# A fused attention and mixing kernel: one exponential, two folds and a division change places at the end of the attention stage

## What is computed

```
def phi(x):
    proj = np.einsum('bhsd,df->bhsf', x, w_phi)
    proj = proj - np.max(np.abs(proj), axis=-1, keepdims=True)
    return np.concatenate([np.exp(proj), np.exp(-proj)], axis=-1)
q_p, k_p = (phi(q), phi(k))
kv = np.einsum('bhsf,bhsd->bhfd', k_p, v)
z = np.sum(k_p, axis=2)
num = np.einsum('bhsf,bhfd->bhsd', q_p, kv)
den = np.einsum('bhsf,bhf->bhs', q_p, z)[..., None] + 1e-06
return (num / den).astype(np.float32)
```

```
X = np.fft.fft(x, axis=1)
X = np.fft.fft(X, axis=2)
mixed = np.real(X).astype(np.float32)
u = x + mixed
...
ch = np.maximum(un @ w_ch1, 0.0) @ w_ch2
return (u + ch).astype(np.float32)
```

## Time and profile before

| | |
|---|---|
| time, median of 3 (lowest to highest) | 1013.8 us (1013.75 to 1014.8) |
| time of the profiled execution | 1013.84 us |
| its span, first to last instruction | 1012.0 us |
| mean granted clock of TensorE | 0.989 of full |
| busy: TensorE / VectorE / ScalarE / GpSimd | 1001.8 / 654.7 / 557.3 / 364.6 us |
| attention and transform, until the perceptron has TensorE alone | about 272 us |

### The profile page before, as it was taken

How to read it: one execution, slowest core, us unless ns; L and a number is a source line. 1 busy time by engine, 2 the same in 40 slices (tenths; PEclk the granted TensorE clock), 3 DMA queues, 4 the chain that set the end, 5 groups by cost and what they waited for, 6 DMA issues and landing times.

```text
span 1012.0 us, 16785 instructions
## 1 busy us (share of the span) xinstructions
PE 1001.8 (99%) x5866; PEld 928.5 (92%) x5866; DVE 654.7 (65%) x1156; ACT 557.3 (55%) x1018; POOL 364.6 (36%) x362
## 2 busy tenths in 40 slices
PE   9999999998999999999999999999999999999997
PEld 8999999998999899899999998999999999989996
DVE  6676769887875567565675556846567455765443
ACT  5655555753575555555656656556655566634431
POOL 3633334533252444413533236323272242622110
PEclk9999999996999999999999999999999999999999
DMA  6333132201153223232232331332324322242202
GB/s 181 72 92 90 38 72 54 54 13 33 58 151 105 63 67 105 66 99 83 64 94 67 90 104 45 91 95 69 99 63 136 104 67 90 63 141 67 63 2 63
DMA packets 101313, 80.31 MB, mean 79 GB/s; under 512 B 56944, under 2 KB 81776, under 8 KB 101232
## 3 DMA queue, kind: packets, MB, share of 16 engines
q1 hardware_dynamic: 100992, 78.91, 28.0%
q10 hardware_dynamic: 240, 0.33, 0.1%
HBM read 66.10 MB, written 4.72 MB: 70 GB/s over the span
## 4 chain that ended last, share of the span: by engine, by line
PE 95%; DVE 3%; issue 1%; ACT 0%; DVEq 0%; ACTq 0%
PE bank L1180 39%; PE bank L1157 35%; PE bank L408 6%; PE bank L421 5%; PE bank L374 3%; PE bank L660 2%; PE bank L680 2%; PE bank L392 1%; PE bank L426 1%; PE bank L368 1%; DVE shift_k L483 0%; DVE xall L544 0%; PE bank L331 0%; DVE amax_k L470 0%; DVE xn L1515 0%
## 5 line engine op out<-in xcount | busy, mean ns | idle before, releaser
L1180 PE MATMUL bank<-w2op,hid 128*128 128x512 f32 x1728 | 423.2, 390 | 0.0
L1180 PEld LDWEIGHTS bank<-w2op,hid 128*128 128x128 f32 x1728 | 321.6, 188 | 53.4 <-issue 0.3
L1157 PE MATMUL bank<-x_T,w1op 128*128 128x384 f32 x1152 | 208.1, 335 | 0.0
L1157 PEld LDWEIGHTS bank<-x_T,w1op 128*128 128x128 f32 x1152 | 201.2, 188 | 3.9
L1157 PE MATMUL bank<-x_B,w1op 128*128 128x384 f32 x864 | 173.5, 336 | 0.0
L1157 PEld LDWEIGHTS bank<-x_B,w1op 128*128 128x128 f32 x864 | 154.4, 188 | 11.4
L1351 POOL TENSOR_TENSOR w_sums<-st_w 128x256 f32<-128x256 f32 x48 | 49.3, 1028 | 224.4 <-DVE w1op L1387 224.4
L1467 DVE SCALAR_TENSOR_TENSOR hid<-part_s,hid 128x384 fp32r<-128x384 f32 x141 | 98.2, 723 | 37.7 <-ACT hid L1463 37.6
L1408 DVE TENSOR_TENSOR w2op<-st_w,w2op 128x1024 fp32r<-128x1024 f32 x48 | 62.7, 1306 | 45.9 <-ACT w2op L1404 45.9
L1319 POOL TENSOR_TENSOR x_sums<-xraw 128x256 f32<-128x256 f32 x30 | 22.3, 764 | 194.5 <-ACT xraw L1272 124.4
L1463 ACT ACTIVATE hid<-part_s 128x384 fp32r<-128x384 f32 x141 | 73.3, 524 | 31.2 <-DVE part_s L1437 31.2
(11 more groups left out here) (181 smaller groups left out, 1508.7 us busy)
## 6 DMA issues: line engine op xcount, KB each, us to landing
st_w<-w1a SPq DMA_DIRECT2D x24, 512.0 KB, 3.4
st_w<-w2a SPq DMA_DIRECT2D x24, 512.0 KB, 3.6
st_w<-w1b SPq DMA_DIRECT2D x24, 512.0 KB, 3.4
st_w<-w2b SPq DMA_DIRECT2D x24, 512.0 KB, 3.6
v<-v SPq DMA_DIRECT2D x16, 256.0 KB, 3.9
out<-xall SPq DMA_DIRECT2D x16, 256.0 KB, 2.1
rawqk<-qkT SPq DMA_DIRECT2D x14, 288.0 KB, 4.1
rawqk<-qkT SPq DMA_DIRECT2D x14, 256.0 KB, 3.6
```

Of the source, the lines that this page charges most:

```text
L1157: last = nc.tensor.matmul(dst, w1op[g % 2][:, a, W1OP.index(w), c, :], xop[x][:, b, c, :], start=name in ("M2", "M1", "M7") and k_ == 0, s ...
L1180: last = nc.tensor.matmul(acc[t0 + t][:, :], hid[name, g % 2][:, x, P * t:P * (t + 1)], w2op[g % 2][:, y, j, :], start=first and k_ == 0, ...
```

## The change

Three things.

1. **TensorE.** In `pe_unit`, the waits for the two parts of q and k (`qk_hi`, `qk_lo`) stood ahead of all five units of a pair. They now stand ahead of units 0 and 2 alone, with the same values. Units 1, 3 and 4 drop theirs, two each, in slots 2 to 15.
2. **ScalarE.** In slot 15 the two roundings of batch 3's folds move behind the exponential of k. Behind slot 15, the two row copies of batch 2 (`act_place288`) move behind the exponentials of q of pair 15.
3. **VectorE.** In slot 15 the two folds move ahead of the last two pairs of sums of batch 2, and their second parts move out of the slot, behind the first half of pair 14's division.

```diff
@@ pe_unit
-        pe.wait_ge(qk_hi, 2 * (g - 2) + (1 if u < 2 else 2))
-        pe.wait_ge(qk_lo, 2 * (g - 2) + (1 if u < 2 else 2))
+        if u in (0, 2):
+            pe.wait_ge(qk_hi, 2 * (g - 2) + (2 if u else 1))
+            pe.wait_ge(qk_lo, 2 * (g - 2) + (2 if u else 1))
         unit_free(pe, g, u)
@@ dve_slot, g == PAIRS - 1
             dve_features(dve, g, 1)
+            dve_fold_odd(dve, *f_)
+            dve_fold_even(dve, *f_)
             dve_sumdiff(dve, b_, 1)
             dve_sumdiff(dve, b_, 2)
-            dve_fold_odd(dve, *f_)
-            dve_fold_even(dve, *f_)
-            dve_fold_lo(dve, *f_, True)
-            dve_fold_lo(dve, *f_, False)
             return
@@ act_slot
-        if g == PAIRS - 1:
-            act_fold_hi(act, *f_, True)
-            act_fold_hi(act, *f_, False)
@@ behind the slots, ScalarE
             l = PAIRS - 1
-            act_place288(act, B - 2)
+            act_fold_hi(act, B - 1, 0, True)
+            act_fold_hi(act, B - 1, 0, False)
             for r in range(ROUNDS):
                 act_exp_qT(act, l, r)
+            act_place288(act, B - 2)
             act_x_hi(act, 0, 0)
@@ behind the slots, VectorE
             dve_finish(dve, l - 1, 0)
+            dve_fold_lo(dve, B - 1, 0, True)
+            dve_fold_lo(dve, B - 1, 0, False)
             dve_first_sum(dve, "T2", xblock("B22"), xsum("T1", 0))
             dve_finish(dve, l - 1, 1)
```

## The result

The changed kernel takes **1003.1 us** (median of four executions, 1002.03 to 1004.11) against 1013.88 of the kernel before in the same comparison (1013.75 to 1014.8): a ratio of 0.9892, 95% interval 0.9875 to 0.9909. The forecast was 1004.7, with a range from 1003.0 to 1010.2.

What follows compares the result with a forecast made beforehand. TensorE was taken as the bound, with a 3.05 us wait ahead of pair 15's k'v that also halved its clock. Gain 9.4 at S1 less 0.3 behind it is 9.1 off 1013.84: 1004.7 us, range 1003.0 to 1010.2.

Steps and rivals of the forecast that it cites:

- The first wait: TensorE ahead of pair 15's k'v, held by pair 14's division: the 3.05 us are gone.
- The stall in k'v: Middle of pair 15's k'v, waiting for the second half of pair 14's division: a new stall of 1.0 us.
- The stall ahead of S1: TensorE ahead of transform S1, waiting for VectorE to finish pair 15's division: a stall of 2.2 us.
- T4 on VectorE: VectorE behind pair 14's division: ready at 235.3, waits for GpSimd's third addition, ends 0.81 after it, at 237.45.
- rival (c): Pair 14's division also waits for GpSimd through the shared ports: everything 1.5 later, 1006.2 us; chance 0.02.
- The exponential and the row copies: ScalarE: exponential of k ends near 229.2, no longer holding TensorE; row copies behind exponentials of q' end at 235.0.
- (b): The clock falls in the 1.0 us stall in k'v, narrow matmuls behind it: gain 3.9, 1009.9 us; chance 0.12.
- (a): The clock falls in the 2.2 us stall ahead of S1, losing 2.1: 1006.8 us; chance 0.20.
- (d): Pair 14's division stays behind something unseen and releases k'v near 235: no gain, 1013.8 us; chance 0.06.
- (e): Slower: the clock falls at the first stall and S1's stall breaks up the work that restores it; chance 0.04.
- Fewer waits on TensorE: Units 1, 3 and 4 of 14 pairs drop two waits each: costed at 0, at most 0.5 gained.

Runs made afterwards that it cites:

- the kernel with 0.5 us more of wait: The changed kernel with the folds' second parts moved behind the second half of pair 14's division as well: 1003.49 us, ratio 0.9904 to the kernel before.
- the filled wait: The kernel before with 13 identity matmuls between pair 15's transposes and its k'v, nothing else changed: 1003.7 us, ratio 0.9907.

## Why the prediction was right, and where it was not

**The first wait and VectorE's order.** Right, with the 0.75 of the start taken off every forecast time: the exponential ends at 228.5 (forecast 228.4), the first half of the division at 231.1 (231.05), the blocked L762 at 232.3 (232.3), the second half's row at 233.66 (233.7), S1 at 247.5 (247.3). The stall in k'v is 0.7 for 1.0, since the first 18 records took 2.12 and not 1.93 and the division came 0.1 sooner. The stall ahead of S1 is 2.2 as forecast. One reading was off, with nothing resting on it: a quarter at 0.56 puts the clock's fall at 234.78, 2.2 us behind TensorE's last matmul, and not at 234.86 and 2.3.

**One step was wrong and did no harm.** "T4 on VectorE, ready at 235.3, waits for it and ends 0.81 after as before." T4 started at 234.42, 0.11 before GpSimd's addition, and took 0.95. Instead the addition took 2.33 for 1.64, the two x_B second parts behind it took 2.39 and 2.14, and pair 15's division began at 241.65 against a forecast of 241.6. Who goes first changed; the sum of the work on both engines did not.

**The ports.** The four L545 ran in 1.15 from 229.99, beside L827 (228.65 to 230.29) and L817 from 230.25. They were not blocked, so rival (c) is out: the row with a PSUM source in the earlier trace rows was the right guide. The section of the Trainium skill that the prediction names there (SBUF — State Buffer, Who interferes with whom) gives tensor_scalar as an operation that can contend when its operands meet conditions set out elsewhere; that these four would wait was the prediction's own step, and the trace speaks against it.

**The exponential and the row copies.** I let ScalarE's part take its place in the sum without asking what the change would be without it. Alone it gives nothing, and within the change it costs 0.8 to 0.9, through the row copies. The forecast had the later additions in it, but as a given.

**The rivals.** (b), a fall in the stall of k'v, was not seen in any of the traces, eight of which have that wait of 0.7. (a) is the likely reading of part of the executions: 2 of the first 4 are near 1004 at a clock of 0.998, and the kernel with 0.5 us more of wait has that mean in all four. It was put 2.1 us above the forecast; the executions at 0.998 are 1.6 to 2.2 above those near 1002.3. They are why the median is 1003.1 and not 1002.2. (d) and (e) did not occur.

**The term that failed.** "Fewer waits on TensorE: ... No idle stands at them in the view of the waits ... I cost them at 0, and at most at 0.5 gained." They gained **2.05 us**, over a fifth of the forecast gain, and none of it where they stand. The reading of the waits was right and answered another question: 42 instructions fewer on TensorE took away a 16 KB fetch from under the last store. The sum with this term, 1004.7 - 2.05 = 1002.65, and with the start's 0.75, 1001.9, is within 0.15 of the profiled 1002.03. Three of the four experiments with the old waits have ends of 5.4 to 5.9 for 3.55, 1.8 to 2.4 us more; in the fourth, the filled wait, the fetch had moved ahead of the last matmul.

**Open.** Why the 67th matmul comes between 14.2 and 15.5 us, and so which of two otherwise equal executions is a microsecond faster. Why a wait of 1.8 or 2.2 lets the clock fall in one execution and not in the next; none of the slower executions of the change itself was caught by the profile, so that they are rival (a) rests on their mean clock and on the neighbour kernel that shows it, and two of the five (at 1.000 and at 0.949) don't fit it.

## What to carry to other kernels

A short wait of TensorE ahead of narrow matmuls is to be priced by the clock that it may lose, here 7.8 us for a wait of 3; fill it with dummy matmuls as a first test, which takes one line and tells at once whether the clock or the wait is the cost. Look at the end of the trace as its own stage: compare last matmul to end of span, and look for an instruction fetch beside the last store, since here 42 instructions fewer, or 26 matmul records more, moved it out from beside the store. And take a change that has several parts apart, even one that wins: the part on ScalarE cost 0.9 us of what the part on VectorE brought.

## What the runs showed of the hardware

- **An instruction fetch beside the last store goes with an end that is 2 us longer.** A packet of 16 KB took 0.9 to 1.8 us, and 17 or 18 packets of the store left late (ends of 5.4 to 5.9 us in four traces, 3.54 to 3.56 in ten without such a fetch).
- **For waits in between, the clock falls in some executions and not in others of one kernel.** By mean granted clock, with the wait taken from the profile of each kernel: ahead of k'v, waits of 3.0 lost it in all 64 executions whose clock is listed (three kernels) and 1.8 in 8 of 10; ahead of S1, 2.7 lost it in 4 of 4, and 2.2 (the change, and the change with its waits back) by the mean clock in 5 of 17, at 0.998 or 0.997, with the one at 0.949 not counted; 1.3 and less have no clear case. The two places differ in the work around them, so their figures are no one scale. Once down, it stayed down for 17.07 or 20.48 us under the narrow matmuls of k'v and q'kv (TensorE busy 14.00 of 14.00 us at 0.50, above), but only 3.41 us under the transform and the perceptron's products.
- **VectorE and GpSimd, both inputs in SBUF: the one that starts second waits.** L1293, started inside an addition, ended 0.81 behind it twice (235.28 + 2.39 against 234.53 + 2.33; 237.84 + 2.14 against 236.82 + 2.35). T4 and T2, started 0.11 and 0.01 before an addition, took 0.95 and 0.94, and the additions 2.33 and 2.42 for 1.64. The page SBUF — State Buffer (section Who interferes with whom) of the Trainium skill says that issue order decides who blocks, and the traces agree. A lead of 0.01 us was enough to decide it.
